# An attention, convolution and MLP kernel: tails of inputs and outputs transposed in one use of the bank, first loads issued from two queues, key-value sums copied ahead of the weights, the third part of w_out loaded sooner

## What is computed

```python
# attention: 8 heads of 64, 128 random features of both signs
def phi(x):
    proj = x @ w_phi
    proj = proj - max(abs(proj), axis=-1)
    return concat(exp(proj), exp(-proj))
kv  = phi(k).T @ v                     # per head, over the 576 tokens
out = (phi(q) @ kv) / (phi(q) @ sum(phi(k)) + 1e-6)
# gated convolution: d_model 512, d_ff 1024
h    = relu(x @ w_in)
conv = sum over 3 taps of conv_w[k] * h shifted by k - 1 tokens
x    = (h * sigmoid(conv)) @ w_out
# mixer: tokens through rank 32, channels through 2048
u   = x + (x.T @ U @ V).T
out = u + relu(u @ w_ch1) @ w_ch2
```

## Time and profile before

| | |
|---|---|
| median of three runs | 932.11 us (931.59 to 932.53) |
| time of the profiled execution | 931.04 us |
| its span, first to last instruction | 929.2 us |
| TensorE (PE) busy | 900.5 us, 97% |
| weight load (PEld) busy | 834.3 us, 90% |
| VectorE (DVE) busy | 377.8 us, 41% |
| ScalarE (ACT) busy | 326.5 us, 35% |
| GpSimd (POOL) busy | 90.9 us, 10% |
| chain that ended last | PE 85%, DVE 4%, SP's queue 4%, DMA 3%, issue 2%, ACT 1% |
| granted TensorE clock, mean | 0.995 of full |

### The profile page before, as it was taken

How to read it: one execution, slowest core, us unless ns; L and a number is a source line. 1 busy time by engine, 2 the same in 40 slices (tenths; PEclk the granted TensorE clock), 3 DMA queues, 4 the chain that set the end, 5 groups by cost and what they waited for, 6 DMA issues and landing times.

```text
span 929.2 us, 14087 instructions
## 1 busy us (share of the span) xinstructions
PE 900.5 (97%) x5752; PEld 834.3 (90%) x5752; DVE 377.8 (41%) x655; ACT 326.5 (35%) x621; POOL 90.9 (10%) x60
## 2 busy tenths in 40 slices
PE   6899999999999999999998999999999999999997
PEld 4667889887988889889998999999999999999997
DVE  5455477226774355652595543221211122122111
ACT  5665565334653444543443332111211211211111
POOL 3323022000120001110042001010010010010000
PEclk9899999999999999999999999999999999999999
DMA  7986641304722236114356540110200300300101
GB/s 177 265 229 159 195 143 39 114 17 152 225 51 65 77 102 228 46 46 160 114 191 201 168 124 20 57 46 1 73 30 1 100 3 2 101 1 23 47 1 34
DMA packets 106032, 88.91 MB, mean 96 GB/s; under 512 B 61041, under 2 KB 92657, under 8 KB 103921
## 3 DMA queue, kind: packets, MB, share of 16 engines
q1 hardware_dynamic: 105968, 88.02, 31.6%
HBM read 70.18 MB, written 17.83 MB: 95 GB/s over the span
## 4 chain that ended last, share of the span: by engine, by line
PE 85%; DVE 4%; SPq 4%; DMA 3%; issue 2%; ACT 1%; ACTq 0%
PE qnb L1067 7%; PE qnb L1069 7%; PE qnb L1068 7%; PE qnb L1163 7%; PE mb L1067 6%; PE kvb L1124 6%; PE pjb L1067 5%; PE mb L1069 5%; PE mb L1068 5%; PE pjb L1069 5%; PE pjb L1068 5%; PE tpb L1067 2%; PE kvb L1069 2%; PE kvb L1067 2%; PE tpb L1068 2%
## 5 line engine op out<-in xcount | busy, mean ns | idle before, releaser
L985 DVE SCALAR_TENSOR_TENSOR c_lo<-qnb,c_hi 128x384 fp32r<-128x384 f32 x94 | 52.4, 558 | 284.9 <-ACT c_hi L752 284.9
L752 ACT ACTIVATE c_hi<-qnb 128x384 fp32r<-128x384 f32 x94 | 46.3, 492 | 296.6 <-PE qnb L1069 296.6
L1067 PE MATMUL qnb<-u_hi,w_b 128*128 128x384 f32 x384 | 129.8, 338 | 0.0
L1069 PE MATMUL qnb<-u_hi,w_b 128*128 128x384 f32 x384 | 128.4, 334 | 0.0
L1068 PE MATMUL qnb<-u_lo,w_b 128*128 128x384 f32 x384 | 128.4, 334 | 0.0
L809 DVE TENSOR_REDUCE nm<-pjb 128x4 f32<-128x512 f32 (+1 forms) x80 | 50.7, 633 | 84.5 <-PE pjb L1069 84.3
L508 POOL TENSOR_TENSOR g_lo<-cv,g_hi 128x576 fp32r<-128x576 f32 x32 | 48.2, 1505 | 361.5 <-DVE g_hi L794 361.5
L1067 PE MATMUL mb<-x_hi,winr 128*128 128x288 f32 x224 | 72.3, 323 | 0.1
L1067 PEld LDWEIGHTS qnb<-u_hi,w_b 128*128 128x128 f32 x384 | 72.1, 188 | 0.1
L1068 PEld LDWEIGHTS qnb<-u_lo,w_b 128*128 128x128 f32 x384 | 72.1, 188 | 0.0
L1069 PEld LDWEIGHTS qnb<-u_hi,w_b 128*128 128x128 f32 x384 | 72.1, 188 | 0.0
(11 more groups left out here) (257 smaller groups left out, 1929.2 us busy)
## 6 DMA issues: line engine op xcount, KB each, us to landing
winr<-wi_dram SPq DMA_DIRECT2D x32, 512.0 KB, 4.6
woutr<-wo_dram SPq DMA_DIRECT2D x15, 1024.0 KB, 5.9
stage<-in_moe_w_ch_dram SPq DMA_DIRECT2D x32, 256.0 KB, 4.6
us<-u_dram SPq DMA_DIRECT2D x6, 768.0 KB, 4.7
ua<-u_dram SPq DMA_DIRECT2D x6, 768.0 KB, 4.8
kr<-in_k_dram SPq DMA_DIRECT2D x32, 128.0 KB, 3.0
qr<-in_q_dram SPq DMA_DIRECT2D x32, 128.0 KB, 2.7
vt<-in_v_dram SPq DMA_DIRECT2D x32, 128.0 KB, 2.9
```

What stands on the lines that cost most here:

```text
L752: nc.scalar.activation(c_hi[:, j % CR, :], CH[j % 2][:, 0:TW], ACT.Relu).then_inc(s_chh, 1)
L985: nc.vector.scalar_tensor_tensor(out=c_lo[:, j % CR, :], in0=CH[j % 2][:, 0:TW], scalar=0.0, in1=c_hi[:, j % CR, :].bitcast(F32), op0=ALU. ...
L1067: mm(o, a_hi, b_hi, start=start, stop=False)
L1069: return mm(o, a_lo, b_hi, start=False, stop=stop)
```

## The change

Five edits stand in it:

- `T_TAIL` goes from -1 to -3, which is place 2 as well. The tails of the inputs of pair g and the tail of the output of pair g - 3 (`TAILS` = 3) are transposed in one use of `TP`, into columns 0 to 127 and 128 to 191. Place 4 has no use of the bank any more. PE, ACT and DVE do both halves in that use, and SP's tail loads move with it.
- The first loads: SP issues the query tails, the keys of one head, the queries; ACT's queue issues, ahead of its table load, the key tails, the keys of the other head and the two copies of w_phi. The tails are transposed first, in tick -3.
- On ACT, `key_values` stands ahead of `prepare_high`; on PE, `kv_by_feature` behind `project`.
- The third part of w_out is loaded at m 12 in place of 13.
- At the end of the attention: the first two token tiles' loads `us` and `ua` are issued between the last loads of w_in and no longer behind the store of the third batch; the last gate's low part is made by DVE and not by POOL; `hidden2(1, 2)` stands ahead of the wait for the last sums of the mixing.

```diff
     BATCH = PERIOD * PAIRS
-    T_K, T_TAIL, T_Q, T_OUT, T_OUTT = -2, -1, 1, 10, 12
+    T_K, T_TAIL, T_Q, T_OUT, T_OUTT = -2, -3, 1, 10, 12
...
+    TAILS = (T_OUTT - T_TAIL) // PERIOD
     K0, K1, TL, Q0, Q1 = range(PERIOD)
...
     MLP0 = PERIOD * (PAIRS - 1) + T_OUTT + 1
-    FIRST = T_K
+    FIRST = T_TAIL
     END = PERIOD * (NP - 1) + CQ0 + 2
...
     def tp_use(tick):
-        for kind, offset in (("o", T_OUT), ("q", T_Q), ("p", T_OUTT), ("k", T_K), ("t", T_TAIL)):
-            if here(tick, offset) is not None and (kind, here(tick, offset)) != ("p", NP - 1):
+        for kind, offset in (("o", T_OUT), ("q", T_Q), ("k", T_K)):
+            if here(tick, offset) is not None:
                 return kind, here(tick, offset)
-        return None
+        n, i = divmod(tick - T_TAIL, PERIOD)
+        return ("t", n) if i == 0 and 0 <= n < NP - 1 + TAILS else None
...
-        return TPN["p" if b < B - 1 else "o", PAIRS * b + PAIRS - 1]
+        last = PAIRS * b + PAIRS - 1
+        return TPN["t", last + TAILS] if b < B - 1 else TPN["o", last]
...
-            load_k(0)
+            load_tail(0, QROWS, qd)
+            load_k(0, 0)
             for h in range(2):
-                sp.dma_start(ph_raw[h * D:(h + 1) * D, :], w_phi).then_inc(s_phi_ld, 16)
-            load_tail(0)
+                load_q(0, h)
             sp.wait_ge(s_zero, 2)
-            load_q(0)
             load_v(0)
...
                         load_wout(b, m - 2)
-                    if m in (13, 14):
-                        load_wout(b, m - 11)
+                    if m in (12, 14):
+                        load_wout(b, m // 2 - 4)
...
                     sp.wait_ge(s_tp, TPN["k", g] + 1)
-                    load_k(g + 2)
+                    for h in range(2):
+                        load_k(g + 2, h)
                 g = here(tick - 1, T_TAIL)
...
                     sp.wait_ge(s_tp, TPN["t", g] + 1)
-                    load_tail(g + 2)
+                    load_tail(g + 2, QROWS, qd)
+                    load_tail(g + 2, KROWS, kd)
                 g = here(tick - 1, T_Q)
...
                     sp.wait_ge(s_tp, TPN["q", g] + 1)
-                    load_q(g + 2)
+                    for h in range(2):
+                        load_q(g + 2, h)
                 g = here(tick - 1, 4)
...
                 load_win(B - 1, j)
+                if j == J1 - 3:
...
+                    sp.wait_ge(s_xl, len(TPN))
+                    sp.wait_ge(s_ust, 16 * (B - 2))
+                    load_u(us, s_us, 0)
+                    load_u(ua, s_ua, 0)
             sp.wait_ge(s_u, 2 * CC * (B - 1))
             sp.dma_start(u_dram[:, :, (B - 2) * S:(B - 1) * S], x1[:, :, :]).then_inc(s_ust, 16)
...
-            sp.wait_ge(s_xl, len(TPN))
-            sp.wait_ge(s_ust, 16 * (B - 1))
-            load_u(us, s_us, 0)
-            load_u(ua, s_ua, 0)
             for n in range(SLOTS):
...
             last.then_inc(s_const_rdy, 1)
-            for n in range(J1 * B):
+            for n in range(J1 * B - 1):
                 gate_low(n)
...
                 if kind == "t":
-                    act.wait_ge(s_pj, max(0, PERIOD * (g - 1) + TL + 1))
-                    copy(xl_hi[:, :], TP[:, 0:P]).then_inc(s_xh, 1)
+                    if g < NP:
+                        act.wait_ge(s_pj, max(0, PERIOD * (g - 1) + TL + 1))
+                        last = copy(xl_hi[:, :], TP[:, 0:P])
+                    if g >= TAILS:
+                        last = copy(x0_hi[:, (g - TAILS) % XS, MAIN:S], TP[:, P:P + TAIL])
+                    last.then_inc(s_xh, 1)
                 if kind == "q":
...
                     last.then_inc(s_xh, 1)
-                if kind == "p":
-                    copy(x0_hi[:, g % XS, MAIN:S], TP[:, 0:TAIL]).then_inc(s_xh, 1)
...
+            kd = k.rearrange("b (c h) s d -> b c h s d", h=2)
+            act.dma_start(tl[KROWS, 0, :, :],
+                          kd[0, 0, :, MAIN:S, :].rearrange("h s d -> s h d")).then_inc(s_tld[0], 16)
+            act.dma_start(kr[:, 0, :, 1, :],
+                          kd[0, 0, 1, 0:MAIN, :].rearrange("(p t) d -> p t d", t=TM)).then_inc(s_kld[0], 16)
+            for h in range(2):
+                act.dma_start(ph_raw[h * D:(h + 1) * D, :], w_phi).then_inc(s_phi_ld, 16)
             act.wait_ge(s_ident, 1)
...
                 mlp(b, m, 1)
+                g = here(tick, 4)
+                if g is not None:
+                    key_values(g)
                 for n in range(NA):
...
                         prepare_high(n)
-                g = here(tick, 4)
-                if g is not None:
-                    key_values(g)
                 if 0 <= m < J1:
...
                 dve.wait_ge(s_xh, TPN[kind, g] + 1)
-                n = {"t": P, "p": TAIL}.get(kind, MAIN)
-                hi, lo = {"k": (xk_hi, xk_lo), "q": (xq_hi, xq_lo), "t": (xl_hi, xl_lo)}.get(kind, (None, None))
+                if kind in "kq":
+                    hi, lo = (xk_hi, xk_lo) if kind == "k" else (xq_hi, xq_lo)
+                    last = sub(lo[:, :], TP[:, :], hi[:, :].bitcast(F32))
                 if kind == "o":
-                    hi, lo = x0_hi[:, g % XS, 0:MAIN], x0_lo[:, g % XS, 0:MAIN]
-                elif kind == "p":
-                    hi, lo = x0_hi[:, g % XS, MAIN:S], x0_lo[:, g % XS, MAIN:S]
-                else:
-                    hi, lo = hi[:, :], lo[:, :]
-                last = sub(lo, TP[:, 0:n], hi.bitcast(F32))
-                if kind == "o" and g == NP - 1:
-                    last = sub(x0_lo[:, g % XS, MAIN:S], KVT[:, 0:TAIL], x0_hi[:, g % XS, MAIN:S].bitcast(F32))
+                    last = sub(x0_lo[:, g % XS, 0:MAIN], TP[:, :], x0_hi[:, g % XS, 0:MAIN].bitcast(F32))
+                    if g == NP - 1:
+                        last = sub(x0_lo[:, g % XS, MAIN:S], KVT[:, 0:TAIL], x0_hi[:, g % XS, MAIN:S].bitcast(F32))
+                if kind == "t":
+                    if g < NP:
+                        last = sub(xl_lo[:, :], TP[:, 0:P], xl_hi[:, :].bitcast(F32))
+                    if g >= TAILS:
+                        slot = (g - TAILS) % XS
+                        last = sub(x0_lo[:, slot, MAIN:S], TP[:, P:P + TAIL], x0_hi[:, slot, MAIN:S].bitcast(F32))
                 last.then_inc(s_xl, 1)
...
                     gate_high(b, j - 1)
+                if j == J1:
+                    dve.wait_ge(s_gh, J1 * B)
+                    sub(g_lo[:, J1 - 1, :], cv[:, (J1 * B - 1) % HR, :],
+                        g_hi[:, J1 - 1, :].bitcast(F32)).then_inc(s_glast, 1)
                 if j == 0:
...
                 if kind == "t":
-                    pe.wait_ge(s_tld[g % 2], 32 * (g // 2 + 1))
-                    last = nc.tensor.transpose(TP[:, 0:P], tl[:, g % 2, :, :].rearrange("p h d -> p (h d)"),
-                                               ident[:, :])
+                    if g < NP:
+                        pe.wait_ge(s_tld[g % 2], 32 * (g // 2 + 1))
+                        last = nc.tensor.transpose(TP[:, 0:P], tl[:, g % 2, :, :].rearrange("p h d -> p (h d)"),
+                                                   ident[:, :])
+                    if g >= TAILS:
+                        last = nc.tensor.transpose(TP[:, P:P + TAIL], at[QROWS, (g - TAILS) % 2, TM, :],
+                                                   ident[QROWS, QROWS])
                 if kind == "o":
...
                         last = nc.tensor.transpose(KVT[:, 0:TAIL], at[QROWS, g % 2, TM, :], ident[QROWS, QROWS])
-                if kind == "p":
-                    last = nc.tensor.transpose(TP[:, 0:TAIL], at[QROWS, g % 2, TM, :], ident[QROWS, QROWS])
                 last.then_inc(s_tp, 1)
...
                         pe.wait_ge(s_wo[c % 2], woutr_loads(b, c))
-                if e == 0:
+                if e == 0 and (b, last) == (B - 1, J1):
+                    pe.wait_ge(s_gl, J1 * B - 1)
+                    pe.wait_ge(s_glast, 1)
+                elif e == 0:
                     pe.wait_ge(s_gl, J1 * b + last)
...
                 mlp(b, m, 1)
-                g = here(tick, KVT0)
-                if g is not None:
-                    kv_by_feature(g)
                 g, u = unit_at(tick)
...
                     project(g, u)
+                g = here(tick, KVT0)
+                if g is not None:
+                    kv_by_feature(g)
                 use = tp_use(tick)
...
                 hu(b, 1, w, HUB[1][w])
+            hidden2(1, 2)
             pe.wait_ge(s_u, 2 * CC * B)
             for j in range(J2):
-                if j > 1:
+                if j > 2:
                     hidden2(1, j)
```

40 lines of the change are left out of this document (20 added, 20 removed).

## The result

| | before | after |
|---|---|---|
| median | 931.85 us (4 runs, 930.87 to 932.53) | 919.28 us (4 runs, 919.14 to 919.40) |
| profiled execution | 931.04 us | 919.22 us |
| its span | 929.2 us | 917.4 us |
| mean granted clock | 0.995 | 1.000 |

After over before is 0.9866, 95% interval 0.9849 to 0.9883. Not all of its terms hold, as the experiments show.

A forecast was written before the change was run, and what follows sets the result against it. PE, busy 97% of the span, was taken to bound the kernel, leaving only its waits to win. Gains of 3.1 + 2.4 + 2.4 + 3.2 = 11.1 us gave 919.9 from the profiled 931.04, forecast as 921.0 us; range 917.5 to 926.0.

The forecast's parts named there:

- Part 1: First loads and order of tails and keys: PE's keys' transposition waits for the tails' low part; costs 1.9 us.
- my upper bound: At the start: queries issued from the other queue push w_phi back by 1 us, and the cost is 3 us.
- Part 2: Ticks 9 and 10: copying key-value sums ahead of weights removes the 2.5 us gap and low clock; gains 3.1 us net.
- ahead of the weights on ACT: Tick 9: ACT's key-value copy done at 38.6, before the 2.04 us weights' copy, so PE does not wait on it.
- The 0.8 us of waiting forecast for tick 10: Before the query features' second half: PE waits 0.8 us for ACT's exponentials, too little to expect the clock to fall.
- Part 3: One use of the transposition bank per period instead of two, removing place 4's wait; gains 2.4 us.
- the 1.1 that I had: Bank gaps in two periods holding convolution work: all 1.1 us goes, as other matmuls lie between.
- Part 4: w_out's third part, issued sooner, lands before PE asks; both gaps go, gaining 2.4 us.
- Part 5: End of the attention: waits on w_out's last part, the gate's low part and the mixing's sums shrink; gains 3.2 us.
- ACT remains the bound in ticks 9 and 10: Rival: late stores put exponentials back, the clock still falls and part 2 is lost: 924.1 us; chance 15%.
- DMA throughput: Rival: waits of parts 4 and 5 are throughput, not issue; half of 5.6 us returns, about 925; chance 9%.
- The double use of the bank: Rival: keys' transposition in place 3 comes late behind place 2's copies and subtractions, making 935.4 us; slower, chance 2%.

The follow-up runs named there:

- experiment 1: The changed kernel, with ACT copying the weights' part ahead of the key-value sums again, PE's order staying changed: 917.70 us.
- Experiment 7: The changed kernel, with DVE taking the first tails' low part ahead of its wait for w_phi: 917.57 us.
- 2: The changed kernel with both key-value orders undone: weights ahead of sums on ACT, transposed sums ahead of the projection on PE: 917.83 us.
- 5: The kernel before with only the tails' transpositions merged and moved, with their loads; every other part of the change undone: 927.23 us.
- experiment 10: The changed kernel with the third part of w_out loaded at m 13 again: 923.16 us.
- experiment 11: The changed kernel with all three end-of-attention edits undone (mixing loads behind the last store, last low part on POOL, hidden2(1, 2) behind the wait): 924.07 us.
- 9: The changed kernel with DVE's first tails' low part ahead of w_phi, ACT's weights ahead of sums, and SP's constants loaded in tick 14: 915.83 us.

## Why the prediction was right, and where it was not

- **Part 1, the start, -1.9.** The mechanism was right: the keys' transposition waits for the tails' low part, which waits for w_phi. The size was taken at the row's own landing; w_phi came 0.8 us later, so the keys' transposition starts at 7.71 and not at 6.9, and the first projection 2.35 us later than before. That is the case of my upper bound in a milder form; that the queries beside it push w_phi back is not shown, only that it comes later where two queues are used. Of the 2.9 us lost by 24.9 us, 0.7 are not of this part: experiment 1 wins them back in tick 5, by the order on ACT. Experiment 7 shows that 2 us were a matter of DVE's order and not of the merging.
- **Part 2, key-value order, +3.1 net.** Together with part 1 it came out at +1.8 by 46.4 us, or +4.7 gross in its own stretch against 5.0. The gap and the low clock went, as forecast, but the step "ahead of the weights on ACT" is the one that failed as a cause. Experiments 1 and 2 show the gap gone without it, and 917.70 us without it for 919.28 with it. What removed the gap is PE's later arrival, which with the merged use alone leaves 1.1 us of it (5), and SP's four fewer issues, which let the stores land before ACT needs them and leave 0.23 (2). I had weighed the second queue at nothing for w_phi, rightly, and not asked what SP's later issues gain by it, though I had named the stores as what ended the wait. I also priced tick 9 alone: in tick 4 the same order put the exponentials behind the weights, and PE's wait of 1.46 us at 26.16 costs 0.67 us more than with the old order. No term of my sum had it. The 0.8 us of waiting forecast for tick 10 was 0.68, but it was a cost of the new order and not what is left when it has done its work: experiment 1 has none there.
- **Part 3, the bank, +2.4.** Pair-only periods gave 1.1 for the 1.3 worked out (0.2, 0.4 and 0.5), with a wait for the normalised output of 0.28 us each, where I had said 0.6. Beside the convolution 4.3 were won in all, of which 2.4 (experiment 10) to 2.9 (the two jumps between the traces) are w_out's; 1.4 to 1.9 are left for the 1.1 that I had. The listed gaps of 0.56 moved rather than vanished (the waits on `xt_lo` at line 1240 grew from 0.2 to 0.5 each). Where the further gain comes from was not taken apart.
- **Part 4, w_out, +2.4.** Right in its mechanism: the wait is gone and comes back when undone. 2.4 to 2.9, since the listed gaps of 2.4 cost a little more than their length.
- **Part 5, the end, +3.2.** 3.9 in the traces, 4.0 by experiment 11. Each stall cost 0.2 to 0.3 us more than the gap that the waits view lists.
- **Rivals.** ACT remains the bound in ticks 9 and 10, yet by its own 2.1 us of weights and not by the landing; the clock did not fall. DMA throughput limits neither w_out nor the last part: both waits went with the issue. The double use of the bank shows no gap at a tails' or keys' transposition behind the second pair.

So 11.1 forecast and 11.8 found in the spans, with -1.0 at the start, +0.8 beside the convolution, +0.7 at the end of the attention and +0.7 behind the last instruction as the larger errors. They are of both signs, and that the sum came out so near is in part luck: one part that costs 1.5 us was counted as a gain of 3.1, and effects that no term had filled its place. The rest of the 12.6 us between the medians is the draw of the kernel before, whose profiled execution was 0.8 below its median.

## What to carry to other kernels

Where a wait ends on a DMA, look at the issuing engine's own row back to the start: if it never pauses, the lever is the number of issues ahead, and one move can make a reordering elsewhere needless or harmful. Before putting a short operation ahead of a long one, see whether the engine would stand idle until the short one's input is there; the long one may fit into that hole. When several edits land together, undo each one by itself: here one of five cost 1.5 us inside a gain of 12.6. And where a row names what ended a wait, check that the instruction waits for it at all: another run in which it starts sooner than the named one ends settles it.

## What was not expected of the hardware

- **The clock's fall behind a gap comes in some executions and not in others, and goes with much of the spread of the times.** Of the gaps of 1.45 us in experiment 11, one trace has the low clock behind it and the other has not; the code up to there is the same, though PE's smaller waits ahead of it differ (0.77 and 0.58 us near 15 and 18 us for one of 0.55). In 23 runs of the kernel before in one series (927.38 to 932.88 us), those with a mean granted clock of 0.999 and 0.998 took 927.38 to 928.47 us, the five with 0.995 took 931.01 to 932.88, and the two with 0.993 took 931.64 and 932.05. The clock does not tell all: in experiment 10 a run with 1.000 took 922.25 us and one with 0.998 took 924.75. The merged use alone ran from 926.12 (clock 1.000) to 932.60 (0.993). Experiments 1, 2 and 9, whose longest gap behind PE's first projection is 0.6 to 0.7 us, spread by 0.09 to 0.16 us. So of the 12.6 us between the medians, up to some 4 (an estimate: 931.85 less about 928) go with the low clock of the kernel before, and the rest with its gaps themselves. The fastest runs of experiments 10 and 11, 921.57 and 923.14, lie 2.3 and 3.9 above the changed kernel's median, which is what their gaps cost; their medians add 1.6 and 0.9.
- **Three runs of a kernel with gaps say little of its spread.** The 0.1% given at the start was that of 931.59 to 932.53 us; the 23 runs spread by 0.6% about a median of 930.25. From that median the gain would be 11.0 us and not 12.6.
- **The end of the span is 0.7 us shorter where ACT's queue had been used at the start.** The last store of the output, issued by SP, lands 3.2 to 3.3 us behind its issue and not 4.0. It is seen in thirteen of thirteen traces; the store before it takes 3.1 to 3.2 in all of them. Why isn't known.
